# Probabilities times v in fp32, two heads on the two column halves of TensorE

## The reference

```python
def _attn_ref(q, k, v, f):
    scores = scale * np.matmul(q, k.transpose(0, 1, 3, 2))
    log_f = np.log(np.clip(f, 0.0001, 1.0))
    cum = np.cumsum(log_f, axis=-1)
    decay = cum[:, :, :, None] - cum[:, :, None, :]
    scores = np.where(causal, -1000000000.0, scores + decay)
    scores = scores - np.max(scores, axis=-1, keepdims=True)
    attn = np.exp(scores)
    attn = attn / (np.sum(attn, axis=-1, keepdims=True) + 1e-09)
    return np.matmul(attn, v).astype(np.float32)
...
    attn_out = _attn_ref(**attn_kwargs)
    x = np.ascontiguousarray(attn_out.transpose(0, 2, 1, 3)).reshape(B * S, H * D)
    x = _moe_ref(x=x, **moe_kwargs)
    return _moe2_ref(x=x, **moe2_kwargs)
```

## Time and profile before

| what | us |
|---|---|
| median of 3 runs (lowest, highest) | 574.15 (572.37, 575.91) |
| the profiled execution's own time | 575.39 |
| its span | 573.6 |
| TensorE busy | 553.6 |
| VectorE busy | 335.2 |
| ScalarE busy | 297.4 |
| GpSimd busy | 55.7 |

### The profile page before, as it was taken

The page is one execution under the profiler, slowest core; times in us unless marked ns, Lnnn a source line. Parts: engine busy times, 40 slices in busy tenths (PEclk is TensorE's granted clock), DMA queues, the critical chain, the costliest instruction groups (busy, mean ns, idle before and its releaser), DMA issues. The chain is left out here.

```text
span 573.6 us, 9450 instructions
## 1 busy us (share of the span) xinstructions
PE 553.6 (97%) x3634; PEld 501.7 (87%) x3634; DVE 335.2 (58%) x667; ACT 297.4 (52%) x590; POOL 55.7 (10%) x66
## 2 busy tenths in 40 slices
PE   7798999999899999999999999999999999999995
PEld 3486777778799999999999999989999899999994
DVE  4656887886845556574746557486643533344342
ACT  4677777763845446373544547366533334333331
POOL 7113111100451000000000000000000200010002
PEclk8989999999999999999999999999999999999999
DMA  5898562520276262634546252254200100001001
GB/s 134 202 275 178 123 197 83 157 74 2 87 246 222 74 220 75 221 111 184 178 167 221 96 221 74 74 150 144 74 1 0 57 0 2 0 18 39 0 1 55
DMA packets 51246, 63.64 MB, mean 111 GB/s; under 512 B 30529, under 2 KB 30561, under 8 KB 51201
## 3 DMA queue, kind: packets, MB, share of 16 engines
q1 hardware_dynamic: 48304, 57.34, 32.5%
q0 software_dynamic: 1520, 4.77, 2.3%
q10 hardware_dynamic: 1376, 0.92, 0.7%
HBM read 58.25 MB, written 4.77 MB: 110 GB/s over the span
## 5 line engine op out<-in xcount | busy, mean ns | idle before, releaser
L284 DVE TENSOR_TENSOR slot<-stage,slot 128x1024 fp32r<-128x1024 f32 x80 | 95.7, 1222 | 19.6 <-ACT slot L277 19.6
L997 ACT ACTIVATE act_t<-ps,half 128x384 f32<-128x384 f32 x48 | 27.9, 581 | 108.9 <-PE ps L790 108.9
L277 ACT ACTIVATE slot<-stage 128x1024 fp32r<-128x1024 f32 x80 | 81.6, 1052 | 1.9 <-DMA stage<-in_moe_w_out_dram 1.9
L1300 DVE SCALAR_TENSOR_TENSOR act_t<-act_t 128x384 f32<-128x384 f32 x48 | 26.8, 558 | 91.1 <-ACT act_t L997 91.1
L728 PE MATMUL ps<-xe,slot 128*128 128x288 f32 x256 | 75.3, 294 | 0.7 <-issue 0.7
L728 PE MATMUL ps<-hid,slot 128*128 128x288 f32 x256 | 75.6, 295 | 0.0
L729 PE MATMUL ps<-hid,slot 128*128 128x288 f32 x256 | 75.6, 295 | 0.0
L729 PE MATMUL ps<-xe,slot 128*128 128x288 f32 x256 | 75.6, 295 | 0.0
L730 PE MATMUL ps<-hid,slot 128*128 128x288 f32 x256 | 75.3, 294 | 0.0
L730 PE MATMUL ps<-xe,slot 128*128 128x288 f32 x256 | 75.3, 294 | 0.0
L958 ACT ACTIVATE hid<-ps 128x288 fp32r<-128x288 f32 x64 | 26.5, 415 | 91.0 <-PE ps L730 89.8
(11 more groups left out here) (170 smaller groups left out, 1048.1 us busy)
## 6 DMA issues: line engine op xcount, KB each, us to landing
stage<-in_moe_w_dram SPq DMA_DIRECT2D x32, 1024.0 KB, 5.3
cb<-c_scratch SPq DMA_DIRECT2D x7, 576.0 KB, 4.1
stage<-in_moe_w_in_dram SPq DMA_DIRECT2D x6, 512.0 KB, 3.8
stage<-in_moe_w_out_dram SPq DMA_DIRECT2D x6, 512.0 KB, 3.7
x_sorted<-x_scratch SPq DMA_DIRECT2D x9, 258.0 KB, 4.5
q_nat<-in_q_dram SPq DMA_DIRECT2D x16, 128.0 KB, 2.7
v_nat<-in_v_dram SPq DMA_DIRECT2D x16, 128.0 KB, 4.3
cb<-c_scratch SPq DMA_DIRECT2D x14, 144.0 KB, 4.4
```

Of the source, the lines that this page charges most:

```text
L277: nc.scalar.activation(s[:, 0, at], stages[n_buf][:, at], ACT.Copy).then_inc(w_hi, 1)
L284: nc.vector.tensor_tensor(s[:, 1, at], stages[stage_of(g)[0]][:, at], s[:, 0, at].bitcast(F32), ALU.subtract).then_inc(w_lo, 1)
```

## The change

- `vs`, and with it GpSimd's splits, are gone, and `pt1` and `pt2` hold plain fp32 without parts. A new tile `spare` (7424 numbers per partition) is allocated and not used.
- The transposed probabilities are only copied: head 0 and the last tile by ScalarE, head 1 by VectorE.
- `times_v` multiplies in fp32: v of one head (64 columns) is the weight, head 0 writes PSUM partitions 0 to 63, head 1 partitions 64 to 127 of the same bank. Both heads stand together: the first part in t = 3, the second part in t = 1.
- `ot` holds the two heads on its two partition halves. One output product per tile has 144 columns (72 per head), five instead of ten, all in t = 3. `rg` has zeros where the heads don't meet. `normalize` works on tiles 0 to 2 and then 3 and 4 of both heads.
- The start: f of the first pair isn't broadcast by DMA. The one scan of 16 rows is done first, and four fp32 products (`spread_sums`) put the first pair's two rows on all partitions, in columns 0 to 255 and then 256 to 575; ScalarE and VectorE copy them into `cb`, and VectorE copies the first k. The spin of eight products ahead of the first score is gone, and in pair 0 the transposes of pair 1's q and k stand one step later. SyncE writes the sums to DRAM ahead of pair 1's loads and loads the decay of pair 1 ahead of pair 2.
- Loads of v wait for the product that read the buffer (`pv_ps`).
- At the end the tiles of both heads are done together, the last one in ten fp32 products instead of twenty fp32r ones.

```diff
 
 
         att = ExitStack()
-        pt1 = sb("pt1", [P, 2, 2, 2, G1], F32R, att)
...
                              ).then_inc(v_in[p % 2], 16)
 
             load_pair(0)
-            sp.wait_ge(f0_in, 16)
+            sp.wait_ge(f_steps, 3)
+            sp.dma_start(c_dram[:, :], fl[:, 0, :]).then_inc(c_out, 16)
             sp.wait_ge(qk_in[0], 112)
             load_pair(1)
             load_v(0)
-            sp.wait_ge(f_steps, 3)
-            sp.dma_start(c_dram[:, :], fl[:, 0, :]).then_inc(c_out, 16)
-            load_pair(2)
             sp.wait_ge(c_out, 16)
             load_decay(1)
+            load_pair(2)
             load_v(1)
             load_chunk(sp, 0)
...
             def probs_t(n):
                 t = n % NT
                 for u, hd in units(n):
                     pe.wait_ge(exped, u + 1)
-                    if freed_by(u):
-                        pe.wait_ge(pt_lo, freed_by(u))
+                    for w in freed_by(u):
+                        copied(w)
...
+            def times_v(p, pt, tiles, q0, q1, b):
+
+                for j in range(tiles):
+                    for hd in range(2):
+                        a = max(Q0[j] - (0 if pt is pt1 else G1), q0)
+                        last = mm(ps[64 * hd:64 * hd + 64, 512 * b + a - q0:512 * b + q1 - q0], v_nat[:, p % 2, j, hd],
+                                  pt[:, hd, j, a:q1], start=(j == 0), stop=(j == tiles - 1))
                 last.then_inc(pv_ps, 1)
...
+            def output_tile(p, t):
+
+                at, b = divmod(t, 3)[::-1]
+                return mm(bank(6 + b, 2 * XC, 2 * XC * at), ot[:, P * t:P * t + P],
+                          rg[:, p % (HEADS // 2)].rearrange("p r c -> p (r c)"), start=True, stop=True)
...
             pe.wait_ge(ones_set, 1)
+            def spread_sums(a, b):
+
+                for hd in range(2):
+                    last = mm(bank(4 + hd, b - a), ident[0:2, hd:hd + 1].to_broadcast([2, P]), fl[0:2, 0, a:b], start=True, stop=True)
+                return last
...
+            pe.wait_ge(f_steps, 3)
+            spread_sums(0, 256).then_inc(c0_ps, 1)
...
-            spin(8, 4)
             score(0)
             score(1)
+            pe.wait_ge(c0_a, 1)
+            pe.wait_ge(c0_v, 1)
+            spread_sums(256, S).then_inc(c0_ps, 1)
...
-                if t == 1:
-                    if p >= 1:
-                        times_v_second(p - 1, 0, 5)
-                    if more:
-                        pe.wait_ge(qk_sb, 2 * (p + 1) + 1)
-                        transposed(p + 1, 1)
-                if t == 2 and p >= 1:
-                    if more:
-                        pe.wait_ge(qk_sb, 2 * (p + 1) + 2)
-                    else:
-                        pe.wait_ge(xl_sb, 2 * (p - 1))
-                    times_v_second(p - 1, 1, 6)
+                if t == 1 and p >= 1:
+                    pe.wait_ge(pt_a, NT * p)
+                    pe.wait_ge(pt_v, LAST * p)
+                    pe.wait_ge(o1_sb, p)
+                    times_v(p - 1, pt2, NT, 0, G2, 5)
+                if t == (2 if p == 0 else 1) and more:
+                    pe.wait_ge(qk_sb, 2 * p + 1)
+                    transposed(p + 1, 1)
                 if t == 3:
                     if p >= 1:
-                        if not more:
-                            pe.wait_ge(o1_sb, 2 * p)
-                        output(p - 1, 0, 7)
-                        pe.wait_ge(o2_sb, 2 * p - 1)
-                    times_v_first(p, 0, 5)
-                if t == 4:
-                    if p >= 1:
-                        output(p - 1, 1, 6)
-                        pe.wait_ge(xl_sb, 2 * p - 1)
-                    else:
-                        pe.wait_ge(qk_sb, 4)
-                    times_v_first(p, 1, 7)
+                        if more:
+                            pe.wait_ge(qk_sb, 2 * p + 2)
+                        else:
+                            pe.wait_ge(xl_sb, 2 * (p - 1))
+                        output(p - 1)
+                    pe.wait_ge(pt_a, NT * p + 2)
+                    pe.wait_ge(pt_v, LAST * p + 2)
+                    pe.wait_ge(v_in[p % 2], 48 * (p // 2 + 1))
+                    times_v(p, pt1, 2, 0, G1, 5)
...
-            pe.wait_ge(pt_lo, UNITS * PAIRS - 1)
+            pe.wait_ge(pt_a, NT * PAIRS - 1)
+            pe.wait_ge(pt_v, LAST * PAIRS)
             pe.wait_ge(maxed, UNITS * PAIRS)
-            times_v_full_tiles(0, 0)
-            times_v_full_tiles(1, 1)
-            for hd in range(2):
-                pe.wait_ge(o1_sb, 2 * end + hd + 1)
-                for t in range(2):
-                    output_tile(end, hd, t, bank(5 + 2 * hd, XC, XC * t))
-            pe.wait_ge(pt_lo, UNITS * PAIRS)
+            times_v(end, pt2, LAST, 0, 2 * P, 0)
...
-            def probs_hi(n, u, hd):
+            def probs_copy(n, u, hd):
                 p, t = divmod(n, NT)
                 act.wait_ge(pt_ps, u + 1)
                 if p >= 1 and t in (0, 2):
-                    act.wait_ge(pv_ps, 4 * (p - 1) + t + hd + 1)
-                A.activation(*probs_pair(n, u, hd, 0), ACT.Copy).then_inc(pt_hi, 1)
-
-            def copy_second(p, hd):
-                act.wait_ge(pv_ps, 4 * p + 3 + hd)
-                A.activation(ot[:, hd, G1:S], bank(5 + hd, G2), ACT.Copy).then_inc(o2_sb, 1)
-
...
-                    if i < len(old):
-                        probs_hi(n - 1, *old[i])
+                    if i == 0 and old:
+                        probs_copy(n - 1, *old[0])
...
+            V.tensor_tensor_scan(fl[:, 0, :], ones[0:BH], fl[:, 1, :], 0.0, ALU.mult, ALU.add).then_inc(f_steps, 1)
+
+            def first_sums(a, b):
+
+                dve.wait_ge(c0_ps, 1 if a == 0 else 2)
+                V.tensor_copy(cb[:, 0, 1, a:b], bank(5, b - a)).then_inc(c0_v, 1)
+
+            first_sums(0, 256)
+            dve.wait_ge(qk_ps, 2)
+            for a, b in ((0, 256), (256, S)):
+                V.tensor_copy(k_t[:, 0, a:b], bank(2, b - a, a)).then_inc(k0_sb, 1)
...
-            def probs_lo(n, u, hd):
-                dve.wait_ge(pt_hi, u + 1)
-                to, src = probs_pair(n, u, hd, 1)
-                V.tensor_tensor(to, src, probs_pair(n, u, hd, 0)[0].bitcast(F32), ALU.subtract).then_inc(pt_lo, 1)
-
-            def copy_first(p, hd):
-                dve.wait_ge(pv_ps, 4 * p + 1 + hd)
+            def probs_copy(n, u, hd):
+                p, t = divmod(n, NT)
...
+            def normalize(p, part):
+                ts, n = (slice(0, 3), 3) if part == 0 else (slice(3, NT), 2)
+                dve.wait_ge(ox_ps, 2 * p + part + 1)
                 dve.wait_ge(r_inv, 3 * p + 3)
-                V.tensor_tensor(xl[:, 2 * p + hd], bank(7 - hd, XC * NT).rearrange("p (t c) -> p t c", t=NT),
-                                rinv[:, p % 2, hd, :].unsqueeze(2).to_broadcast([P, NT, XC]), ALU.mult).then_inc(xl_sb, 1)
+                V.tensor_tensor(xl[:, 2 * p:2 * p + 2, ts, :].rearrange("p h t c -> p t h c"),
+                                bank(6 + part, 2 * XC * n).rearrange("p (t h c) -> p t h c", t=n, h=2),
...
-                if n >= 1:
-                    for u, hd in units(n - 1):
-                        probs_lo(n - 1, u, hd)
+                if n >= 1 and (n - 1) % NT < LAST:
+                    probs_copy(n - 1, *units(n - 1)[1])
```

More of the change, by code:

```diff
@@ L547, in probs_t @@
                     last.then_inc(pt_ps, 1)
-            def times_v_first(p, hd, b):
-                pe.wait_ge(pt_lo, UNITS * p + 3 + hd)
-                pe.wait_ge(v_lo, p + 1)
-                for part in range(2):
-                    for j in range(2):
-                        last = mm(bank(b, G1 - P * j, P * j), vs[:, p % 2, hd, j].rearrange("p x d -> p (x d)"),
-                                  pt1[:, hd, part, j, P * j:G1], start=(part == 0 and j == 0), stop=(part == 1 and j == 1))
-                last.then_inc(pv_ps, 1)
@@ L677, in _ @@
+            for t in range(2):
+                output_tile(end, t)
+            pe.wait_ge(pt_a, NT * PAIRS)
+            times_v(end, pt2, NT, 2 * P, G2, 1)
+            pe.wait_ge(o2_sb, PAIRS)
+            output_tile(end, 2).then_inc(ox_ps, 1)
+            output_tile(end, 3)
             pe.wait_ge(o_last, 1)
-            pe.wait_ge(r_inv, 3 * PAIRS)
-            for hd in range(2):
-                last = output_tile(end, hd, LAST, bank(2, XC, XC * hd))
-            last.then_inc(ox_last, 1)
+            output_tile(end, LAST).then_inc(ox_ps, 1)
@@ L1112, in _ @@
                             AX_X, ALU.add).then_inc(r_first, 1)
[L1113 to L1120 removed]
+            for part in range(2):
+                normalize(end, part)
             steps = [0]
```

220 lines of the change are left out of this document (102 added, 118 removed).

## The result

| | before | after |
|---|---|---|
| median, us (runs; lowest, highest) | 573.67 (4; 572.37, 575.91) | 567.01 (4; 565.35, 568.12) |
| profiled execution, us | 575.39 | 565.35 |
| its span, us | 573.6 | 563.5 |
| mean granted clock of TensorE in it | 0.992 | 0.997 |

The ratio after to before is 0.987, 95% interval 0.984 to 0.990: faster by 1.3%, 6.7 us. I had forecast 572.8 and no change. A second profile of the same kernel, run later (`after_again`), has a median of 566.5 (4 runs) and a ratio of 0.986 (0.982 to 0.990).

A forecast was written before the change was run, and what follows sets the result against it. TensorE, busy 97% of the span, was taken to bound the kernel. Middle +0.7, start +0.4 and tail -2.5 gave -1.4 against the profiled 575.39, so 574.0, or 572.8 on the median's scale; range 567 to 583.

The forecast's parts named there:

- The price of the products of v: Probabilities times v, per pair of heads: second part 2.30 us, first 0.94, together 3.24 instead of 3.80.
- the fixed 0.21: Per fp32 group: 0.21 us for loads and changing into and out of halves, besides 1.66 ns per column.
- The rule against it: Skill's rule: loads overlap products only where row groups differ, so column halves' loads lie bare; 0.21 a group by the rows.
- the rival of bare loads: Column halves' weight loads not covered: 0.7 to 1.5 us more a pair, 0.5 in the tail; 580, chance 0.17.
- Steps: One pair, score start to score start, beginning at the 512-column score: five steps summing to 14.62 us against 14.65.
- the whole middle stretch: Restart in pair 2 to the last score: -0.15 over five pairs, +0.86 in three last steps, +0.7 us in all.
- The tail: Last score to first routing step: 11.2 us instead of 13.67, so -2.5.
- The start: Up to the restart in pair 2: -1.2 from earlier loads, +1.6 from half clock, +0.4 us in all.
- the restart in pair 2: TensorE resuming after waiting for decay 2: at 44.0 instead of 45.24, set by DMA, after standing 3.2 us.
- The half clock behind the wait (+1.6): After the 3.2 us wait in pair 2: TensorE at half clock for 3.4 us, costing 1.6.
- Decay 2 lands well earlier and the clock stays: Rival at the start: -3 us and no half-clock cost of 1.6, giving 568 to 569; chance 0.10.
- The rival of freer maxima: Waits for maxima don't grow because VectorE is freer: -1.2 us in each of 6 pairs, 566; chance 0.05.

The follow-up runs named there:

- one_half: Changed kernel with both heads' products of v on column half 0, one after the other, into the same 64 partitions: 587.47 us, ratio 1.024.
- split: Changed kernel with key tiles 2 to 4 of the second part of probabilities times v moved in front of the last score: 560.59 us, ratio 0.977.
- before_warm: Kernel before with twelve more idle TensorE products at the start, while it waits for k: 573.93 us, ratio 0.998.
- f_broadcast: Changed kernel with a broadcast of f, its values unused, put back at the head of ScalarE's queue: 573.32 us, ratio 0.998.
- pv_only: Changed kernel with the old start, so only the fp32 products of v and their output are new: 570.08 us, ratio 0.992.
- start_only: Kernel before with the new start alone, products of v and output as they were: 573.56 us, ratio 0.998.
- start_warm: start_only with five more idle TensorE products, two ahead of the spread products and three ahead of the first score: 569.79 us, ratio 0.992.

## Why the prediction was wrong

**The price of the products of v was right.** Forecast 2.30 and 0.94 for the two parts, measured 2.21 (85.36 to 87.57) and 0.80 (94.18 to 94.98). 2.21 less the fixed 0.21 is 1.64 ns per column, where the rows of the row halves gave 1.66. The output took 1.32 (92.86 to 94.18), forecast 1.28. The 0.07 to 0.09 a group that I put on top did not show.

**The rule against it did not hold here.** By the trace, the loads of these products are 137 ns at the median (the line of the products of v, 80 to 96; 31 of the loads are recorded):

```profile
L561 PEld LDWEIGHTS ps<-pt,v_nat x31: 132/137/137, 79.9 to 94.7; 128*64 128x64 f32 x31
```

Twenty of them are 2.7 us, more than the whole 2.21 in which they and the products ran. So the loads, all of them on the same rows, are covered. Nor is it the column halves that cover them: in `one_half` all 20 records use the same rows and the same columns, and 4.25 less the fixed 0.21, over 2432 columns, is again 1.66 ns per column. The Trainium skill (TensorE: Matmul & The Clock Gate, "The mechanism", under "What overlaps and what doesn't") lets a load overlap only where the row group differs. The sentences above that list in the same section add a second case, a load into the background weight buffer, which the prediction left out. The measurement decides, and the rival of bare loads (580) is out.

**The order made of it what was forecast.** Steps, forecast and measured: 2.75 and 2.76; 4.05 and 3.96; 1.43 and 1.52; 2.17 and 2.15; 4.22 and 4.19; a pair 14.62 and 14.58. The saved work did turn into a wait in front of each last score (0.96 idle, 1.2 forecast), and `split` shows that another order of the same products takes it away. Over the whole middle stretch the forecast was +0.7 without the clock, and the measurement -0.84. Five periods took 72.37 instead of 73.79: -1.42 against -0.15, since each is on average 0.15 shorter than forecast (14.47 for 14.62; the pair above is one of the longer ones) and the first of before was the 0.5 longer that I had left out knowingly. The last three steps took 8.14, forecast 8.42.

**The tail was right**: 10.99, forecast 11.2.

**The start is the step that failed**: the restart in pair 2 came 6.7 us sooner where 1.2 were forecast. Beside `before_warm`, which has the old start and full clock up to its restart (42.85), it is 4.3 sooner. It failed at its first number. "f lands near 5.7" is about when the broadcast of f lands in the trace of before (issued at 0.74, 5.1 to landing; f's rows behind it, issued at 1.22, take 5.2), and the change removes exactly that broadcast. Without it f landed at 3.2, and its sums were ready at 5.96 instead of the 8.5 forecast; `f_broadcast` puts the broadcast back, and the sums go out at 9.36.

The first chunk of weights follows these sums. From their write to that chunk SyncE issues one transfer behind the other without a stop, 14.24 us in the changed kernel (5.96 to 20.20) and 14.23 in `f_broadcast` (9.36 to 23.59), though TensorE is at half clock there for most of it (it is 14.69 in `after_again`). So the 2.5 us by which the sums were mis-sized went straight into the first chunk: 1.2 sooner forecast, 3.4 measured (20.20 for 23.56). The rest was priced at nothing: the way from that chunk to decay 2 got 1.5 shorter (7.69 instead of 9.22) and the time from decay 2's issue to the restart 1.8 (10.65 instead of 12.46, the longest landing of cb between 26 and 48 being 8.7 instead of 10.7). 3.4, 1.5 and 1.8 are the 6.7. Some 2.4 of that go with the half clock of before, as said above.

The first score had a second error beside it: 12.7 forecast, 9.03 measured. From the spread products to the first score it takes 2.95 (6.08 to 9.03), where the forecast leaves 4.2 behind its 8.5. And I had tied the restart to the queue alone, with TensorE's own work ready at 40.8. It was ready at 37.8, and decay 2 held it by 0.71.

**The half clock behind the wait (+1.6) did not come in this profile**: the wait was 0.71 and not 3.2. The mechanism exists: `pv_only` has a wait of 2.82 at that place, and half clock from 42.9 to 46.3 right behind it; that pair takes 15.94 us, in the changed kernel 14.38, which is 1.56 more.

```profile
42.59 1.00 PE L520 MATMUL ps<-k_t,q_t 64*128 64x256 f32 x4 [2.82 <-DVE nmax L1009]
```

So a later decay 2 would have cost about what I said. What I left out is that the old start pays half clock of its own in many runs, and that a shorter start can save or lose it: 3.8 us between `start_only` and `start_warm`. At nearly the same clock the change is 5.3 to 6.5 us better than forecast. About 3.1 of that is the restart (4.3 less 1.2), 1.6 the half clock that did not come, and 1.5 the middle stretch.

**The rivals.** "Decay 2 lands well earlier and the clock stays" (568 to 569, chance 0.10) is what came true, and by more than its price of 3 us. I held against it that three chunks still stand ahead; they do, but all four transfers were issued earlier, and decay 2 took 2 us less to land. The rival of freer maxima (566) did not come true, the wait of 0.96 being there. It is what took the range down to 567, so it is luck that the measured 567.0 lies on the range's edge.

## What to carry to other kernels

A landing time read from a trace holds only with the transfers that were in front of it there: when the change removes one, price the landing anew, from the first small transfers of the trace, and follow it through every queue that waits for its consumer. Work that is saved in a step bound by a loop of two engines turns into a wait; look then for work that can be moved into that step, which here was worth as much (6.4 us) as the whole change. Half clock at the start can take as much as a change brings (3.3 to 3.8 us between `start_only` and `start_warm`), and it can come in one kernel and stay away in its neighbour, so compare variants at the same mean granted clock before dividing a gain among parts.

## What the runs showed of the hardware

- fp32 products of 128 rows and 64 columns on the two column halves run at the same time: 20 records in 2.21 us, against 4.25 on one half. Their loads, 137 ns each, are covered in both cases (1.64 and 1.66 ns per column behind the fixed 0.21).
- A broadcast of two rows of 576 numbers to 128 partitions, at the head of a queue, delayed all first loads: f's rows landed 5.2 us after their issue instead of 2.5 (the longest landing of xl in either trace), and the 128 KB loads of q and k of the first pair 5.1 instead of 3.1 and 3.0 (medians, `f_broadcast` and the changed kernel).
- One kernel (`start_only`) had half clock from 11.5 to 18.3 in its profile and a mean clock of 0.985 in most of its runs; the changed kernel had none there, though TensorE stood no less in it: for 0.39 and 0.61 us in the first 9 us, against less than 0.1 and 0.61. Five idle products removed it. What makes the difference between the two kernels stays open: both have their first two scores at 9.03 and 10.34.
- Expert and dense layers take 389.64 us of TensorE's time in the 390 us from 160 to 550 in both kernels: a shift of attention's end is passed on whole.
